# First unit of the expert layer issued ahead of the last two groups of the dense layer's output product, with earlier token loads and splits

## The reference

```python
# attention with a decaying state: per head, state 48x48, 768 steps, 4 batches, 8 heads
state = f[:, :, t, :, None] * state + k[:, :, t] (outer) v[:, :, t]
y[:, :, t] = q[:, :, t] @ state
# dense layer on 3072 tokens x 384, d_ff 2048
h = x @ w_in
g = h * sigmoid(1.702 * h)
x2 = g @ w_out
# four experts, d_ff 1024 each
for e in range(4):
    out += p[:, e:e+1] * (relu(x2 @ w1[e]) @ w2[e])
```

## Time and profile before

| what | value |
|---|---|
| median of 3 runs | 1424.93 us (1424.27 to 1424.94) |
| the profiled execution, its own time | 1423.43 us |
| its span, first to last instruction | 1421.7 us |
| PE busy | 1392.5 us (98%) |
| DVE, ACT, POOL busy | 916.3, 569.0, 626.3 us |
| mean granted TensorE clock | 0.996 |

### The profile page before, as it was taken

The page is one execution under the profiler, slowest core; times in us unless marked ns, Lnnn a source line. Parts: engine busy times, 40 slices in busy tenths (PEclk is TensorE's granted clock), DMA queues, the critical chain, the costliest instruction groups (busy, mean ns, idle before and its releaser), DMA issues.

```text
span 1421.7 us, 20981 instructions
## 1 busy us (share of the span) xinstructions
PE 1392.5 (98%) x8092; PEld 1316.1 (93%) x8092; DVE 916.3 (64%) x1376; ACT 569.0 (40%) x975; POOL 626.3 (44%) x719
## 2 busy tenths in 40 slices
PE   7899999999999999999999999999999999999999
PEld 6799999999999999998999999999999999999998
DVE  7785847566675757346666666666666666666666
ACT  5563534444444535245323332333333333343331
POOL 8776555555473747356412121212212354344430
PEclk9999999999999999999999999999999999999999
DMA  9535243342516051032010010101011111322111
GB/s 155 108 96 75 68 54 84 43 95 32 106 20 118 11 94 35 3 106 72 23 34 28 18 34 23 32 14 34 12 34 52 38 34 58 99 67 67 45 56 45
DMA packets 239796, 79.00 MB, mean 56 GB/s; under 512 B 188752, under 2 KB 238160, under 8 KB 239696
## 3 DMA queue, kind: packets, MB, share of 16 engines
q1 hardware_dynamic: 239696, 77.66, 24.0%
HBM read 67.83 MB, written 9.78 MB: 55 GB/s over the span
## 4 chain that ended last, share of the span: by engine, by line
PE 91%; POOL 2%; DVE 2%; ACT 2%; issue 1%; SPq 1%; DMA 1%; POOLq 0%; ACTq 0%; DVEq 0%
PE bank L1757 9%; PE bank L1755 9%; PE bank L1756 9%; PE bank L1705 8%; PE bank L1706 8%; PE bank L1704 8%; PE bank L1576 6%; PE bank L1668 4%; PE bank L1669 4%; PE bank L1670 4%; PE bank L1504 4%; PE bank L1503 4%; PE bank L1502 4%; PE bank L1608 3%; PE bank L1616 1%
## 5 line engine op out<-in xcount | busy, mean ns | idle before, releaser
L1458 DVE SCALAR_TENSOR_TENSOR acc<-bank,p_n,acc 128x384 f32<-128x384 f32 x384 | 234.7, 612 | 67.4 <-PE bank L1757 62.5
L788 POOL TENSOR_TENSOR g_l<-sig,g_h 128x384 fp32r<-128x384 f32 x128 | 161.2, 1260 | 238.0 <-ACT g_h L1026 238.0
L1757 PE MATMUL bank<-w_h,h_l 128*128 128x384 f32 x768 | 257.2, 335 | 0.0
L1755 PE MATMUL bank<-w_h,h_h 128*128 128x384 f32 x768 | 257.1, 335 | 0.0
L1756 PE MATMUL bank<-w_l,h_h 128*128 128x384 f32 x768 | 256.9, 334 | 0.0
L1442 DVE TENSOR_TENSOR bank<-bank,x_copy 128x512 f32<-128x512 f32 x192 | 124.6, 695 | 164.5 <-ACT x_copy L1126 101.9
L1704 PE MATMUL bank<-xs,we_h 128*128 128x512 f32 x528 | 205.5, 389 | 1.1 <-DVE h_l L1448 1.1
L1706 PE MATMUL bank<-xs,we_l 128*128 128x512 f32 x528 | 206.4, 391 | 0.0
L1705 PE MATMUL bank<-xs,we_h 128*128 128x512 f32 x528 | 206.3, 391 | 0.0
L839 POOL TENSOR_TENSOR we_l<-we_raw,we_h 128x384 fp32r<-128x384 f32 x96 | 96.8, 1033 | 217.1 <-ACT we_h L1092 217.1
L1354 DVE TENSOR_TENSOR sig<-bank,sig 128x384 f32<-128x384 f32 x128 | 71.0, 554 | 176.8 <-ACT sig L1019 175.4
(11 more groups left out here) (145 smaller groups left out, 2577.5 us busy)
## 6 DMA issues: line engine op xcount, KB each, us to landing
we_raw<-in_moe_w SPq DMA_DIRECT2D x32, 384.0 KB, 4.3
w_raw<-in_moe_w SPq DMA_DIRECT2D x32, 384.0 KB, 3.3
v_sb<-in_v SPq DMA_DIRECT2D x24, 192.0 KB, 3.6
x_dram<-work SPq DMA_DIRECT2D x8, 576.0 KB, 3.1
x_raw<-x_dram SPq DMA_DIRECT2D x12, 384.0 KB, 4.0
f_raw<-in_f_logit SPq DMA_DIRECT2D x56, 72.0 KB, 2.1
q_raw<-in_q SPq DMA_DIRECT2D x56, 72.0 KB, 2.1
k_raw<-in_k SPq DMA_DIRECT2D x56, 72.0 KB, 2.0
```

The costliest lines, as they stand in the source:

```text
L788: pool.tensor_tensor(g_l[:, j % RING, :], sig[:, j % 2, :], g_h[:, j % RING, :].bitcast(F32), ALU.subtract).then_inc(gl_ready, 1)
L1458: dve.scalar_tensor_tensor(acc[:, pr * TT + i, :], y_bank[y % 3][:, 0:DM], p_n[:, col:col + 1], acc[:, pr * TT + i, :], ALU.mult, ALU.add) ...
L1755: pe.matmul(dst, hh, wh, start=f == 0, stop=False)
L1757: last = pe.matmul(dst, hl, wh, start=False, stop=f == 1)
```

## The change

It moves code and changes two allocations; no arithmetic is added or left out.

1. TensorE: in `moe`, `first_layer(0)` is called in slot 15, behind layer_out(13) and ahead of layer_out(14) and layer_out(15). Its fifth add waits for the last `gelu_product`, because `sum_b` and `sum_c` are the banks that `hidden` wrote.
2. ACT: x_high(0) in slots 3 to 5 (were 5 to 7), w1_high(0) in slot 6 (was 4), w2_high(0) in slot 7 (was 8), x_high(1) in slots 8 to 10 (were 10 to 12), w1_high(1) in slot 15 ahead of the last gelu_high; x_high(2, 1), x_high(2, 2) and read_x2(7) behind the relus of unit 0 (were ahead of unit 0).
3. DVE: x_sums(0) in slot 2 (was 3), x_low(0) in 4 to 6 (were 6 to 8), x_sums(1) in 8 (was 10), x_low(1) in 9 to 11 (were 11 to 13), x_sums(2) in 14 (was behind the slots); x_low(2, 1) and x_low(2, 2) behind the h_lows of unit 0.
4. POOL: w1_low(1) in slots 15 to 17. Its w1_low(0) stays in slots 5 to 7.
5. SP: store_x2(6) behind load_weights(0) and load_x(0); load_x(0) waits for one store fewer.
6. Memory: x_copy, h_l, h_h in this order, so that unit 0's buffers lie clear of the rows of `wout_h` and `wout_l` that groups 14 and 15 still read.

```diff
@@ memory
+    x_copy = at("x_copy", [P, 3, TB])
+    h_l = at("h_l", [P, 2, 2, 2, TB], F32R)
     h_h = at("h_h", [P, 2, 2, 2, TB], F32R)
-    h_l = at("h_l", [P, 2, 2, 2, TB], F32R)
-    x_copy = at("x_copy", [P, 3, TB])
@@ SP
-            store_x2(HALVES - 2)
...
-            sp.wait_ge(x2_stored, 16 * HALVES)
+            sp.wait_ge(x2_stored, 16 * (HALVES - 1))
             load_x(0)
+            store_x2(HALVES - 2)
             load_x(1)
@@ POOL, moe
-                w1_low(1)
+                    if 15 <= slot < 15 + W1_PARTS:
+                        w1_low(1, slot - 15)
                 clear(0)
@@ ACT, moe
-                    if slot in (5, 6, 7):
-                        x_high(0, slot - 5)
-                    if slot == 4:
+                    if slot in (3, 4, 5):
+                        x_high(0, slot - 3)
+                    if slot == 6:
                         w1_high(0)
-                    if slot == 8:
+                    if slot == 7:
                         w2_high(0)
-                    if slot in (10, 11, 12):
-                        x_high(1, slot - 10)
-                w1_high(1)
-                for part in range(len(X_PARTS)):
-                    x_high(2, part)
-                read_x2(n)
+                    if slot in (8, 9, 10):
+                        x_high(1, slot - 8)
+                    if slot == FT - 1:
+                        w1_high(1)
+                x_high(2, 0)
@@ ACT, units
                 for i in range(1, 4):
                     relu(u, i)
+                if u == 0:
+                    x_high(2, 1)
+                    x_high(2, 2)
+                    read_x2(HALVES - 1)
@@ DVE, moe (x_sums and x_low: slots as listed above)
...
+                    if slot == 14:
+                        x_sums(2)
-                x_sums(2)
                 x_low(2, 0)
-                x_low(2, 1)
@@ DVE, units
-                if u == 0:
-                    x_low(2, 2)
                 sum_of(u, 3, sum_c[:, :], sum_c, 2)
...
+                if u == 0:
+                    x_low(2, 1)
+                    x_low(2, 2)
@@ TensorE (first_layer itself moves up unchanged but for this wait)
                 add(sum_e, s1, t1, True)
+                if u == 0:
+
+                    pe.wait_ge(g_ready, HALVES * FT)
                 add(sum_b, s4, b22, True)
...
             def moe(n):
                 for slot in range(SLOTS):
                     if slot < FT:
                         hidden(n, 1, slot)
                     if slot >= LAG:
                         layer_out(n, slot - LAG)
+                    if slot == FT - 1:
+                        first_layer(0)
...
-            first_layer(0)
             for u in range(1, UX):
```

More of the change, by code:

```diff
@@ L1112, in x_high @@
                 act.activation(x_cols(i, 0, lo, hi), x2_raw[:, lo + 1:hi + 1, :], ACT.Copy).then_inc(x2h_ready, 1)
-            halves_program(alone, both, moe)
             def relu(u, i):
@@ L1126, in copy_x @@
                 act.activation(x_copy[:, i, :], sum_x[:, :], ACT.Copy).then_inc(x_copied, 1)
+            halves_program(alone, both, moe)
             for u in range(UX):
@@ L1419, in moe @@
                     gelu_product(n, slot)
-                    if slot == 3:
+                    if slot == 2:
                         x_sums(0)
-                    if slot in (6, 7, 8):
-                        x_low(0, slot - 6)
-                    if slot == 10:
+                    if slot in (4, 5, 6):
+                        x_low(0, slot - 4)
+                    if slot == 8:
                         x_sums(1)
-                    if slot in (11, 12, 13):
-                        x_low(1, slot - 11)
-                x_sums(2)
+                    if slot in (9, 10, 11):
+                        x_low(1, slot - 9)
+                    if slot == 14:
+                        x_sums(2)
                 x_low(2, 0)
-                x_low(2, 1)
             halves_program(alone, both, moe)
@@ L1684, in both @@
                         layer_out(n, slot - LAG)
[L1686 to L1693, removed]
             def first_layer(u):
@@ L1736, in first_layer, with moe @@
                 add(sum_e, a23, b32, False).then_inc(ff_ready, 1)
+            def moe(n):
+                for slot in range(SLOTS):
+                    if slot < FT:
+                        hidden(n, 1, slot)
+                    if slot >= LAG:
+                        layer_out(n, slot - LAG)
+                    if slot == FT - 1:
+                        first_layer(0)
+            halves_program(alone, both, moe)
             def second_layer(u):
```

## The result

| | before | after |
|---|---|---|
| median | 1425.27 us (1423.98 to 1428.31, 19 runs) | 1428.87 us (1425.66 to 1431.94, 19 runs) |
| profiled execution, its own time | 1423.43 us | 1430.35 us |
| its span | 1421.7 us | 1428.6 us |
| mean granted TensorE clock | 0.996 | 0.994 |

The ratio is 1.0023, with a 95% interval of 1.0015 to 1.0031: the changed kernel takes 3.3 us more (2.1 to 4.4). It is slower, as forecast, and inside the forecast's range.

What follows compares the result with a forecast made beforehand. TensorE, busy nearly the whole span, was taken to bound the kernel. Terms 1.3 + 1.65 + 2.0 = +4.95 us, the 2.5 us gain already counted, gave 1424.93 + 5.0 = 1429.9 us; range 1425.8 to 1431.7.

Steps and rivals of the forecast that it cites:

- the sum: Whole forecast: waits at layer_out(5) and in first_layer(1), then a low clock: 1.3 + 1.65 + 2.0 = +4.95 us.
- The old pauses: TensorE's waits ahead of layer_out(14), 0.96 us, and in first_layer(1), 1.23 us; removing both wins about 2.5 us with restarts.
- TensorE's move: first_layer(0) ahead of layer_out(14) and (15): removes both pauses, its 33 matmuls and the groups' 18 covering POOL and DVE.
- Rival (c): Both old pauses in layer_out(14) and first_layer(1) go, no new one comes: -2.5 us, 1422.4 us; chance 0.09.
- Term 1: Slot 6: POOL's w1_low(0, 0) waits for w1_high(0), delaying gelu_low(5) and TensorE's layer_out(5): +1.3 us.
- Term 2: first_layer(1): late tokens of load_x(3) hold x_high(3, 0) ahead of copy_x(1, 1); TensorE stands 4.0 us, net +1.65 us.
- Term 3: Behind the 4 us pause in first_layer(1) TensorE's granted clock falls to half: +2.0 us, lower bound 0.
- rival (a): Both waits, at layer_out(5) and in first_layer(1), but the clock keeps 2.4 GHz: +3.0, 1427.9 us; chance 0.13.
- (b): load_x(3) lands quickly, so TensorE stands less in first_layer(1): 1426.2 us; chance 0.12.
- (d): As forecast, but w1_low blocked by DVE, load at slow bound, clock low longer: up to +6.9, 1431.8 us; chance 0.06.

Runs made afterwards that it cites:

- e7: Changed kernel, w1_high(0) in slot 4, x_high(3) behind unit 1's relus, x_high(2, 1) and x_low(2, 1) sooner, load_x(3) ahead of store_x2(7); 0.9978 against before.
- e1: The changed kernel with ACT's w1_high(0) moved from slot 6 back to slot 4; timed ratio 1.0022 against the kernel before.
- e2: The changed kernel with the three x_high(3) on ACT put behind unit 1's relus; timed ratio 0.9996 against the kernel before.
- e3: The changed kernel with w1_high(0) in slot 4 and x_high(3) behind unit 1's relus; timed ratio 0.9991 against the kernel before.
- e4: The changed kernel with 14 unused 128x512 matmuls ahead of the ninth add of first_layer(1); timed ratio 1.0025 against the kernel before.
- e6: The changed kernel with ACT's, DVE's and SP's moves of slots 3 to 12 undone; timed ratio 1.0025 against the kernel before.
- e8: The kernel before with the three x_high(3) put behind unit 1's relus; timed ratio 1.0000 against the unedited kernel before.
- e5: The changed kernel with load_x(3) ahead of store_x2(7) on SP; timed ratio 1.0023 against the kernel before.

## Why the prediction was right, and where its sizes were off

The mechanisms were the three of the sum, and the sign followed. The sum was 4.95; the tail shows 3.93 and the timed ratio 3.3.

**The old pauses.** Both went, as the part on TensorE's move said. That they are worth 2.5 us is borne out by e7, which has none of the four pauses and gains 2.27, with 0.1 still lost ahead of first_layer(2). Rival (c), the change as it is meant, asks for this; after fails it at both places that the rival named, the input of w1_low(0, 0) and the take-up of the tokens.

**Term 1** was exact: 1.30, with a wait of 0.97 in the idle column. The bound of 0.7 to 0.8 more didn't come. DVE's x_low(0, 2) ran from 625.91 for 0.95, so to 626.86, and POOL began w1_low(0, 0) at 626.95 and took 1.02. One slot ahead the collision can be seen: x_low(0, 1) and gelu_low(4) started within 0.02 us of each other, and x_low took 1.81, its own 0.95 and most of POOL's 1.01:

```profile
622.71 1.81 DVE L1404 TENSOR_TENSOR xs<-x_raw,xs 128x768 fp32r<-128x768 f32 x1
```

The Trainium skill (SBUF — State Buffer, "SBUF: two separate sides") has it that a DVE operation with two SBUF inputs and a GpSimd one that reads SBUF lock each other out for a whole instruction. The trace agrees, with this 1.81. That it did not meet w1_low(0, 0) was a matter of 0.09 us, so the exactness of Term 1 is in part luck.

**Term 2** was mis-sized. Of the 1.65, 0.15 is the restart, which the rows below count with the nine matmuls; 1.5 is left. In the rows, the ninth add came 1.01 later than Term 1 alone would have it. The load's issue was right: 668.34 less what all was pushed by (4.27) is 664.07, against 664.2. What failed was the chain behind it. x_high(3, 0) came at 669.61 on that axis, not 670.0: the tokens were taken up 5.54 us behind the issue, where I had 5.6 and 0.2 for the store of 576 KB ahead of the load. And copy_x(1, 1) starts 0.74 behind x_high, not 0.85, since ACT's instructions overlap from start to start. The pause came out at 3.2 to 3.4 us, not 4.0, also because TensorE arrived there 0.1 later. The load's time was near the forecast in part by luck. From its issue to POOL's first sum of these tokens, which waits for it in all ten traces, it took 5.58 to 6.13 us with the store right ahead (after, e1, e2, e3, e4, e6) and 5.64, 4.84, 5.15, 4.85 without (before, e8, e5, e7). So the store costs more than the 0.2, and the 5.6 of before that I started from was the slowest of its kind; in after the two errors nearly cancelled. SP's order there is the same in before and e8, and they differ by 0.8, so a single row can't price such a term to better than that.

**Term 3** was right in kind and 0.5 too large: nine matmuls in 3.66 instead of 2.04 is 1.62 with the restart, forecast 2.0 + 0.15. The low stretch of 3.4 us was the shorter of the two rows that I had, and half of it is 1.7; I took 2.0, between 1.7 and 2.4. What could have failed is the fall itself, which I took from a row of 4.54 us: the pause was 3.2, and at 2.65 (e5) there was none. That it came is partly luck: it fell behind all three pauses of over 3.2 us (after, e1, e6), but the length of a pause alone does not decide it (the rows are in the last section). The Trainium skill (TensorE: Matmul & The Clock Gate, "HAM oscillation — how this bites in real kernels") tells of a kernel that waits for a DMA between bursts of matmuls and starts each burst at the low clock. The trace agrees in part: 0.50 behind the 3.22 us, but from 0.4 us into the burst; behind e5's 2.65 us the clock stayed at 1.00.

**The step that was missing** is beside Term 3. I wrote that at half speed DVE has time for its sums of unit 1, and added nothing. That is so in after, where second_layer(0) has no gap. But rival (a), the clock at full speed, was then priced at +3.0 as though the whole term fell away. e4 and e5 show that TensorE at full speed runs into DVE's accumulate and loses 0.57 and 0.59. So the low clock's own cost here is 1.49 - 0.57 = 0.92 us, and rival (a) should have been priced 0.6 higher.

**Rivals.** (a) didn't come: the clock fell. (b), a quick load, didn't: the tokens took 5.54 us. (d) didn't: none of its three bounds was reached.

**Left open.** Why a pause lowers the clock in one execution and not in the next, and so whether after's fall in unit 1 comes in every execution: each kernel has one trace. And why POOL's g_l was late at 194 us in after and not in before.

## What to carry to other kernels

When a change moves the point from which a transfer can be issued, look for every instruction that waits for that transfer and stands ahead of something urgent on its engine: here the gain of 2.5 us was made, and a split that TensorE needed only a unit later turned it into a loss by standing ahead of a copy that it needed at once. Where a low clock or a stall is to be removed, price what runs beside it at full speed too; here the next engine took back 0.6 of 1.5 us. Compare two profiled executions from the last common point ahead of the change, not from the start.

## What the runs showed of the hardware

- **The clock behind a pause.** Behind pauses of 3.22, 3.59 and 3.77 us (idle column; after, e1, e6) the granted clock fell to 0.50, which is 1.2 GHz, not in the pause but some 0.2 to 1.1 us after the matmuls had resumed, and was low for about 3.4 us in each. Behind 2.65 us (e5), and with the pause filled (e4), it stayed at 1.00. I had expected a pause of 4 us to lower it, and had no row between 1.26 and 4.54. But these rows give no bound: the 0.85 us at 194.02 of after lowered it, the 0.97 us at 628.97 did not, and one and the same early pause of 0.58 us went both ways. In e2 (TensorE's row, then a window: length, PE busy, granted clock, DMA share, GB/s):

```profile
202.52 1.99 PE L1609 MATMUL bank<-v_sb,scores_T 128*128 128x48 f32 x16 [0.58 <-DVE state L1340]
```

```profile
205.00:206.00 1.00, 1.00 (x6) 0.52 0.68 78
```

And in before:

```profile
201.70 1.99 PE L1608 MATMUL bank<-v_sb,scores_T 128*128 128x48 f32 x16 [0.58 <-DVE state L1340]
```

```profile
200.00:210.00 10.00, 9.42 (x69) 1.00 0.55 66
```
- **A load's time from issue to use.** The same 384 KB load was taken up by ACT 5.59 and 5.10 us behind its issue with no store right ahead (before, e5), and 5.54, 5.89, 6.01 and 6.08 us with it (after, e1, e4, e6).
- **Executions differ ahead of the change.** The start of read_x2(6) lies between 602.20 and 607.99 us in ten traces. The granted clock goes with it: up to there it was down for 10.2 us in before, e3, e4, e7 and e8 (602.20 to 604.35), for 13.7 in after (606.85), for 17.1 in e1, e2 and e6 (604.45 to 607.99) and for 23.9 in e5 (607.28).
